# Three reordered steps in a gated attention + two-MoE kernel: POOL's weight sums, one DVE accumulation, one PE reduction

## The chip, the cores and the metric

The kernel runs on one core of a Trainium2 chip. The metric is the device time of one execution in microseconds. Engines are named as the profile names them: PE (matmuls), PEld (its weight loads), DVE (VectorE), ACT (ScalarE), POOL (GpSimd), SP (the queue that issues all DMAs here).

## What is computed

The reference has three stages, each feeding the next:

```python
for t in range(S):                                   # gated linear attention, B=2, H=8, S=768, D=48
    state = alpha[:, :, t, :, None] * state + einsum('bhd,bhe->bhde', k[:, :, t], v[:, :, t])
    y[:, :, t] = einsum('bhd,bhde->bhe', q[:, :, t], state)
x = y as 1536 tokens x 384
xn = x / sqrt(mean(x * x) + 1e-6) * rms_g            # first MoE: 384 -> 1536 -> 384
x  = (silu(xn @ w_gate) * (xn @ w_val)) @ w_out
p  = domain_probs / (sum(domain_probs) + 1e-9)       # second MoE: 4 experts, 384 -> 1024 -> 384
out = sum over e of p[:, e] * (relu(x @ w1[e]) @ w2[e])
```

All is fp32. Each product is made of three matmuls over split operands: a "high" half, rounded, and a "low" half, the rest of it: high x high, high x low, low x high.

## The kernel before

**First stage (to about 320 us).** The 1536 tokens go in four quarters of 384 (index i in the code). For each quarter, a list of events (`events()`) is walked by every engine in its own queue order. In the first MoE a quarter has 12 blocks of hidden columns (f = 0 to 11), and the events per block are G (gate product on PE, Silu on ACT), V (value product on PE, the multiplication on DVE at L1215, the high half on ACT at L891, the low half on POOL at L680) and O (output product). Between these, the table `AT` inserts the steps of the next quarter's attention and normalisation, at a position 3 x f + sub with sub 0, 1, 2 for G of f + 1, V of f + 1 and O of f. Of the normalisation: N (position 24; DVE adds up the squares, L1161 and L1163), SS (position 26; PE waits for `s_sqsum`, then sums over partitions with a matmul against ones, L1509; ACT makes `rms` from it, L864, which needs another activation table), R (28; DVE refines `rms`, L1171 to L1177), X (30; DVE scales). DVE takes the low half of the very last block itself (L1219), and then splits the finished activations `x2` into halves (`split_block`, L1009), six blocks and later three more.

**Second stage (from about 320 us).** The hidden columns of all experts go in 16 pairs of 128 (NPAIR = 16). Pair 0 (PLAIN = 1) is computed plainly (`hidden_plain`). Pairs 1 to 15 use a fast scheme with 15 products: POOL makes 11 sums of weight blocks (`sum_first`, L699 to L705, and `sum_second`, L710 to L714), rounds them (`sum_upper`, L721), and takes the low halves (`sum_lower`, L726 and L728, `sum_lower_last`, L733, which sets `s_wu`). DVE and ACT make 11 sums of activation blocks once (`split_sum`, L1238, which counts `s_vl` to 11), and these serve all pairs. PE (`sums_and_outputs`) interleaves the 15 products of a pair (L1606 to L1608, banks A to F) with the 12 output tiles of the pair before (`out_tile`, L1370 to L1372), and DVE combines the banks (L1295), splits them into halves (`split_bank`, L1232) and accumulates each output tile (`add_up`, L1246 for pair 0, L1249 for all others).

**What sets the order around the change.** POOL's buffers: the sums are written to `u_sum`, which nothing else uses at that time; the rounded halves `wuh` and `wul` of pair 2 lie where the plain weights of pair 0 and some of the activation sums lay, and so need `s_plain` = 6 and `s_vl` = 11. POOL's own order at this place: low half of block 10 of the last quarter (L680), then `sum_weights(2)`, then `out_weights(1)` (L674, L676), then `sum_weights(3)`. `sum_first(pair)` of pairs 3 and on waits for the 15 products of the pair before last (`s_mul`). PE waits for `s_wu` = pair before the first product of a pair. On SP, the load of pair 3's first weights waits for `s_wu` = 1, that of pair 2's second weights for pair 1's `out_weights`.

PE's `out_tile` of tile number n (12 per pair) waits for `s_acc` of n - 1, as two banks alternate; tiles 4 and on of a pair need all six banks split (`s_el`). After pair 15's products PE does tiles 9, 10, 11 of pair 14 and tiles 0 to 11 of pair 15, and each finished tile goes out with a DMA (SP).

Of the kernel before, what the change touches and what calls it, by code (L numbers as in the profile page):

```python
# [26 lines left out]
def gated_attention_two_moe(nc, q, k, v, alpha, w_gate, w_val, w_out, rms_g, probs, w1, w2, out):  # L27
    B, H, S, D = q.shape
    DM, FF = w_gate.shape
    E, _, F2 = w1.shape  # L30
    N = B * S
    NP = H // 2
# [11 lines left out]
    with ctx:  # L44
        def sem(name):
            return ctx.enter_context(nc.semaphore(name))
# [99 lines left out]
        NPAIR, PLAIN = E * F2T // 2, 1  # L146
# [12 lines left out]
        V_SUMS = (0, 1, 2, 3, 4, 5, 7, 9, 10, 13, 14)  # L159
# [24 lines left out]
        def nth(order, q, what):  # L184
            return len(order) * q + order.index(what) + 1
# [90 lines left out]
        s_vs, s_vd, s_vh, s_vl = sem("s_vs"), sem("s_vd"), sem("s_vh"), sem("s_vl")  # L276
        s_plain = sem("s_plain")
# [100 lines left out]
        def raw_1(pair):  # L378
            at = pair % 2 * KT * FW
            return stage[:, :, :].rearrange("p a b -> p (a b)")[:, at:at + KT * FW].rearrange("p (j n) -> p j n", j=KT)  # L380
# [11 lines left out]
        STEP = 6  # L392
        PLACES = (("Y", 6), ("T", 0), ("TQ", 1), ("S", 4), ("KV", 5))
        AT = {}
# [3 lines left out]
        for place in AT.values():  # L398
            place.sort(key=lambda step: step[0] != "Y")
        AT[STEP * NP].append(("N", 0))  # L400
        AT.setdefault(STEP * NP + 2, []).append(("SS", 0))
        AT.setdefault(STEP * NP + 4, []).append(("R", 0))
        AT.setdefault(STEP * NP + 6, []).append(("X", 0))
        AT.setdefault(3 * (FT - 2) + 1, []).append(("XS", 0))
# [209 lines left out]
        def _(pool):  # L614
# [70 lines left out]
            def weight_sums(pair):  # L685
                w = {b: both[pair % 2] for b, both in W.items()}
                return w, {m: u_sum[:, n, :] for n, m in enumerate(U_SUMS)}, 3 * (pair - PLAIN)

            def sum_first(pair):
                w, u, _ = weight_sums(pair)  # L690
                if pair == PLAIN + 1:
                    pool.wait_ge(s_vl, len(V_SUMS))
                    pool.wait_ge(s_plain, 6 * PLAIN)
                elif pair > PLAIN + 1:
                    pool.wait_ge(s_mul, 15 * (pair - PLAIN - 1))
                if pair > PLAIN:
                    pool.wait_ge(s_wu, pair - PLAIN)
                pool.wait_ge(s_r1[pair % 2], 16 * (pair // 2 + 1))
                pool.tensor_tensor(u[12], w[1, 1], w[1, 0], ALU.subtract)  # L699
                pool.tensor_tensor(u[8], w[0, 1], w[0, 2], ALU.subtract)  # L700
                pool.tensor_tensor(u[2], w[1, 0], w[0, 0], ALU.subtract)
                pool.tensor_tensor(u[3], w[0, 0], w[0, 2], ALU.add)
                pool.tensor_tensor(u[4], w[0, 0], w[1, 2], ALU.add)
                pool.tensor_tensor(u[10], w[1, 2], w[0, 2], ALU.subtract)
                pool.tensor_tensor(u[11], w[1, 0], w[1, 2], ALU.add).then_inc(s_us, 1)  # L705
# [9 lines left out]

            def sum_upper(pair):
                c, raw, done = pair % 2, raw_1(pair), 3 * (pair - PLAIN)
                pool.wait_ge(s_us, done + 3)
                for rows, src in ((slice(0, NSUM), u_sum), (slice(NSUM, NSUM + 2), raw[:, 0:2, 0:P]),
                                  (slice(NSUM + 2, NU), raw[:, 1:3, P:FW])):  # L720
                    pool.tensor_scalar(wuh[c][:, rows, :], src, 0.0, 1.0, ALU.add, ALU.mult).then_inc(s_uh, 1)  # L721
# [14 lines left out]
            def sum_weights(pair):  # L736
                sum_first(pair)
                sum_second(pair)
                sum_upper(pair)
                sum_lower(pair)  # L740
                sum_lower_last(pair)
# [254 lines left out]
        def _(dve):  # L996
# [232 lines left out]
            def split_hidden(bank, pair, n, f, t):  # L1229
                at = slice(t * TB3, (t + 1) * TB3)  # L1230
                dve.wait_ge(s_eh, 6 * pair + n + 1)
                dve.scalar_tensor_tensor(out=hidl[pair % 2][:, f, at], in0=bank, scalar=0.0,  # L1232
                                         in1=hidh[pair % 2][:, f, at].bitcast(F32), op0=ALU.max, op1=ALU.subtract
                                         ).then_inc(s_el, 1)
# [5 lines left out]
            def add_up(pair, t):  # L1240
                a = acc[:, t * DM:(t + 1) * DM]
                part = full[f"out_ps{t % 2}"][:, 0:DM]
                p = prob_flat[:, t * E + pair // (F2T // 2):t * E + pair // (F2T // 2) + 1]
                dve.wait_ge(s_tile, NTILE * pair + t + 1)
                if pair == 0:
                    dve.tensor_scalar(a, part, p, None, ALU.mult).then_inc(s_acc, 1)  # L1246
                else:
                    dve.wait_ge(s_acc, NTILE * (pair - 1) + t + 1)
                    dve.scalar_tensor_tensor(out=a, in0=part, scalar=p, in1=a, op0=ALU.mult, op1=ALU.add  # L1249
                                             ).then_inc(s_acc, 1)  # L1250
# [40 lines left out]
            for pair in range(PLAIN, NPAIR):  # L1291
                q = pair - PLAIN

                def combine(bank, part, op):
                    dve.tensor_tensor(bank, bank, tcp[part], op).then_inc(s_add, 1)  # L1295

                def split_bank(bank, f, t):
                    split_hidden(full_bank[bank], pair, BANKS.index(bank), f, t)

                dve.wait_ge(s_mul, nth(MULS, q, 13))  # L1300
                dve.wait_ge(s_copy, nth(COPIES, q, 1))
                combine(bank_f, 1, ALU.subtract)
                add_up(pair - 1, 3)
                dve.wait_ge(s_add, nth(ADDS, q, 7))
                dve.wait_ge(s_copy, nth(COPIES, q, 2))
                combine(bank_f, 2, ALU.subtract)
                add_up(pair - 1, 4)
                dve.wait_ge(s_mul, nth(MULS, q, 4))
                dve.wait_ge(s_copy, nth(COPIES, q, 4))
                combine(bank_d, 4, ALU.subtract)  # L1310
                split_bank("F", 1, 2)
                dve.wait_ge(s_mul, nth(MULS, q, 11))
                dve.wait_ge(s_copy, nth(COPIES, q, 8))
                combine(bank_a, 8, ALU.subtract)
                add_up(pair - 1, 5)
                dve.wait_ge(s_mul, nth(MULS, q, 10))
                dve.wait_ge(s_copy, nth(COPIES, q, 7))
                combine(bank_e, 7, ALU.subtract)
                add_up(pair - 1, 6)
                split_bank("A", 1, 0)  # L1320
                add_up(pair - 1, 7)
                dve.wait_ge(s_mul, nth(MULS, q, 2))
                combine(bank_d, 8, ALU.add)
                dve.wait_ge(s_mul, nth(MULS, q, 9))
                combine(bank_c, 0, ALU.subtract)
                dve.wait_ge(s_add, nth(ADDS, q, 3))
                dve.wait_ge(s_copy, nth(COPIES, q, 3))
                combine(bank_c, 3, ALU.subtract)
                split_bank("E", 0, 0)
                add_up(pair - 1, 8)  # L1330
                split_bank("C", 0, 2)
                dve.wait_ge(s_mul, nth(MULS, q, 5))
                dve.wait_ge(s_copy, nth(COPIES, q, 5))
                combine(bank_b, 6, ALU.subtract)
                if pair == NPAIR - 1:
                    add_up(pair - 1, 9)
                dve.wait_ge(s_add, nth(ADDS, q, 8))
                combine(bank_d, 5, ALU.add)
                if pair < NPAIR - 1:
                    add_up(pair - 1, 9)  # L1340
                add_up(pair - 1, 10)
                dve.wait_ge(s_add, nth(ADDS, q, 1))
                dve.wait_ge(s_copy, nth(COPIES, q, 9))
                combine(bank_b, 9, ALU.subtract)
                if pair == NPAIR - 1:
                    add_up(pair - 1, 11)
                split_bank("D", 1, 1)
                if pair < NPAIR - 1:
                    add_up(pair - 1, 11)
                split_bank("B", 0, 1)  # L1350
                add_up(pair, 0)
                add_up(pair, 1)
                add_up(pair, 2)
            for t in range(3, NTILE):
# [3 lines left out]
        def _(pe):  # L1358
# [52 lines left out]
            for name, i, f in events():  # L1411
# [8 lines left out]
                if name in ("T", "TK", "TQ", "AHEAD", "S", "KV", "Y"):  # L1420
                    n = PAIR_ORDER[f]
                    _, k_dm, q_dm, k_sm, sc_sb, banks, y_bank = own_of(i, f)
# [270 lines left out]
```

## Time and profile before

| | |
|---|---|
| median of 3 runs | 701.38 us (701.12 to 702.0) |
| profiled execution: its own time | 698.92 us |
| profiled execution: span, first to last instruction | 697.2 us |
| granted PE clock | 1.000 over the span |
| PE busy | 683.6 us, 98% |
| DVE, POOL, ACT busy | 466.2 us, 329.1 us, 265.3 us |

The profiled execution is 2.5 us below the median of the others; 1.7 us of its own time lie outside the span. A line of the timeline reads: start in us, duration in us, engine, line, operation, out<-in, shape, count if several were merged; in square brackets the time that the engine stood idle before it and who ended that. Matmuls are pipelined, so a matmul of 384 columns "lasts" 0.33 us but the next starts about 0.17 us later, and one of 512 columns about 0.23 us later.

### The profile page before, as it was taken

What the parts mean: (1) busy time and instruction counts of PE and PEld (TensorE: products, weight loads), DVE (VectorE), ACT (ScalarE), POOL (GpSimd) and SP (SyncE); (2) the same over time, 40 slices, a digit from 0 to 9 for tenths busy, and PEclk for the clock granted to TensorE, in tenths of its full rate; (3) what the DMA queues carried; (4) which work ended last, traced back from release to release, by engine and by line L of the source; (5) the groups of instructions that cost most, each with busy time, mean ns of one, the idle gap of its engine ahead of it and who ended that gap; (6) DMA issues with size and microseconds to landing.
All of it is one profiled execution on the core that took longest, in us unless ns stands there. A gap on an engine that the chain in (4) does not pass through costs nothing.

```text
span 697.2 us, 10727 instructions
## 1 busy us (share of the span) xinstructions
PE 683.6 (98%) x3989; PEld 633.9 (91%) x3989; DVE 466.2 (67%) x819; ACT 265.3 (38%) x482; POOL 329.1 (47%) x416
## 2 busy tenths in 40 slices
PE   7899999999999999999989999999999999999998
PEld 6699999999999999998979999999999999999997
DVE  6876657555556543216968777977797778767875
ACT  3932333222522243227534343433344334443430
POOL 3469761111111115770396586457645775577200
PEclk9999999999999999999999999999999999999999
DMA  8995380005102001000011100111011101100003
GB/s 183 225 182 116 98 170 0 9 1 103 35 1 77 1 2 44 3 0 24 1 46 46 47 23 24 46 46 38 9 46 45 46 2 46 46 24 1 23 1 136
DMA packets 71749, 35.14 MB, mean 50 GB/s; under 512 B 53904, under 2 KB 70672, under 8 KB 71696
## 3 DMA queue, kind: packets, MB, share of 16 engines
q1 hardware_dynamic: 71696, 34.44, 19.6%
q8 instruction: 32, 0.52, 0.3%
q14 instruction: 21, 0.17, 0.1%
HBM read 31.48 MB, written 2.36 MB: 49 GB/s over the span
## 4 chain that ended last, share of the span: by engine, by line
PE 88%; DVE 4%; SPq 3%; POOL 2%; ACT 1%; issue 1%; DMA 1%; DVEq 0%; POOLq 0%
PE out_ps L1370 12%; PE out_ps L1372 12%; PE out_ps L1371 12%; PE hid_ps L1363 7%; PE hid_ps L1365 6%; PE hid_ps L1364 6%; PE at_ps L1608 4%; PE at_ps L1607 4%; PE at_ps L1606 4%; PE hid_ps L1607 2%; PE hid_ps L1608 2%; PE hid_ps L1606 2%; SPq L460 2%; PE at_ps L1444 2%; PE at_ps L1458 1%; PE at_ps L1490 1%
## 5 line engine op out<-in xcount | busy, mean ns | idle before, releaser
L1249 DVE SCALAR_TENSOR_TENSOR x<-out_ps,prob,x 128x384 f32<-128x384 f32 x180 | 110.3, 613 | 58.2 <-PE out_ps L1372 58.2
L1371 PE MATMUL out_ps<-early_r,late_r 128*128 128x384 f32 x384 | 129.4, 337 | 0.0
L1370 PE MATMUL out_ps<-early_r,late_r 128*128 128x384 f32 x384 | 129.0, 336 | 0.4 <-DVE x L1249 0.4
L1372 PE MATMUL out_ps<-early_r,late_r 128*128 128x384 f32 x384 | 129.3, 337 | 0.0
L680 POOL TENSOR_TENSOR hid_lo<-act_sb,hid_hi 128x384 fp32r<-128x384 f32 x44 | 44.9, 1020 | 160.9 <-ACT hid_hi L891 160.9
L941 ACT COPY late<-at_ps 128x512 f32<-128x512 f32 x105 | 61.9, 589 | 103.8 <-PE at_ps L1608 100.8
L1215 DVE TENSOR_TENSOR act_sb<-hid_ps,act_sb 128x384 f32<-128x384 f32 x48 | 26.6, 555 | 79.6 <-PE hid_ps L1365 70.2
L1370 PEld LDWEIGHTS out_ps<-early_r,late_r 128*128 128x128 f32 x384 | 72.1, 188 | 6.6 <-DVE x L1249 0.9
L1371 PEld LDWEIGHTS out_ps<-early_r,late_r 128*128 128x128 f32 x384 | 72.0, 188 | 5.6
L1372 PEld LDWEIGHTS out_ps<-early_r,late_r 128*128 128x128 f32 x384 | 72.1, 188 | 0.0
L699 POOL TENSOR_TENSOR early<-stage 128x128 f32<-128x128 f32 x15 | 7.0, 470 | 126.4 <-PE at_ps L1608 98.8
L891 ACT CAST hid_hi<-act_sb 128x384 fp32r<-128x384 f32 x48 | 24.6, 513 | 107.6 <-DVE act_sb L1215 107.6
L1606 PE MATMUL at_ps<-late_r,early_r 128*128 128x512 f32 x135 | 52.5, 389 | 1.8 <-POOL early_r L733 1.8
L1608 PE MATMUL at_ps<-late_r,early_r 128*128 128x512 f32 x135 | 53.6, 397 | 0.0
L1295 DVE TENSOR_TENSOR at_ps<-at_ps,late 128x512 f32<-128x512 f32 x75 | 52.2, 696 | 0.5
L1363 PE MATMUL hid_ps<-xn_hi,wvh 128*128 128x384 f32 x141 | 49.3, 349 | 0.6 <-POOL wvl L610 0.5
L733 POOL TENSOR_TENSOR early_r<-early,early_r 128x1408 fp32r<-128x1408 f32 x15 | 48.5, 3231 | 0.0
L1607 PE MATMUL at_ps<-late_r,early_r 128*128 128x512 f32 x120 | 47.3, 394 | 0.0
L1365 PE MATMUL hid_ps<-xn_hi,wvl 128*128 128x384 f32 x141 | 47.3, 335 | 0.0
L1364 PE MATMUL hid_ps<-xn_lo,wvh 128*128 128x384 f32 x141 | 47.2, 335 | 0.0
L1370 PE MATMUL out_ps<-hid_hi,woh 128*128 128x384 f32 x132 | 46.4, 351 | 0.0
L1363 PE MATMUL hid_ps<-xn_hi,wgh 128*128 128x384 f32 x132 | 46.1, 349 | 0.2 <-DVE act_sb L1202 0.2
(286 smaller groups left out, 1621.5 us busy)
## 6 DMA issues: line engine op xcount, KB each, us to landing
stage<-in_moe_w_dram SPq DMA_DIRECT2D x32, 384.0 KB, 3.5
alpha_all<-in_alpha_dram SPq DMA_DIRECT2D x8, 288.0 KB, 6.2
stage<-in_moe_w_out_dram SPq DMA_DIRECT2D x4, 576.0 KB, 4.0
out_dram<-x SPq DMA_DIRECT2D x12, 192.0 KB, 1.9
stage<-in_moe_w_gate_dram SPq DMA_DIRECT2D x8, 216.0 KB, 3.9
stage<-in_moe_w_val_dram SPq DMA_DIRECT2D x8, 216.0 KB, 4.0
a_tm<-in_alpha_dram SPq DMA_DIRECT2D x9, 192.0 KB, 4.2
k_tm<-in_k_dram SPq DMA_DIRECT2D x9, 192.0 KB, 3.7
```

The source lines that it names most:

```text
L941: act.copy(tcp[n], bank).then_inc(s_copy, 1)
L1249: dve.scalar_tensor_tensor(out=a, in0=part, scalar=p, in1=a, op0=ALU.mult, op1=ALU.add).then_inc(s_acc, 1)
L1295: dve.tensor_tensor(bank, bank, tcp[part], op).then_inc(s_add, 1)
L1363: pe.matmul(dst, ah, bh, start=(n == 0), stop=False)
L1364: pe.matmul(dst, ah, bl, start=False, stop=False)
L1365: mm = pe.matmul(dst, al, bh, start=False, stop=(n == last))
L1370: pe.matmul(dst, ah, bh, start=first, stop=False)
L1371: pe.matmul(dst, ah, bl, start=False, stop=False)
L1372: return pe.matmul(dst, al, bh, start=False, stop=last)
L1606: pe.matmul(bank, ah, bh, start=first, stop=False, skip_group_check=True)
L1607: pe.matmul(bank, ah, bl, start=False, stop=False, skip_group_check=True)
L1608: pe.matmul(bank, al, bh, start=False, stop=True, skip_group_check=True).then_inc(s_mul, 1)
```

## The change

Three things move; no instruction is added and none is taken away.

- The SS event goes from position 26 to 27, so on PE the matmul of L1509 comes after the gate product of block 10 and not before it; on ACT `rms` comes after that block's Silu. It applies to the SS of quarters 1 to 3.
- The two waits of pair 2 (`s_vl`, `s_plain`) go from the start of `sum_first` to the start of `sum_upper`. POOL may make pair 2's 11 sums as soon as it is through with pair 1's and block 10.
- In the last pair, DVE accumulates tile 0 (`add_up(15, 0)`) between the split of bank D and the split of bank B, no longer after both.

```diff
-        AT.setdefault(STEP * NP + 2, []).append(("SS", 0))
+        AT.setdefault(STEP * NP + 3, []).append(("SS", 0))
...
             def sum_first(pair):
                 w, u, _ = weight_sums(pair)
-                if pair == PLAIN + 1:
-                    pool.wait_ge(s_vl, len(V_SUMS))
-                    pool.wait_ge(s_plain, 6 * PLAIN)
-                elif pair > PLAIN + 1:
+                if pair > PLAIN + 1:
                     pool.wait_ge(s_mul, 15 * (pair - PLAIN - 1))
...
             def sum_upper(pair):
                 c, raw, done = pair % 2, raw_1(pair), 3 * (pair - PLAIN)
+                if pair == PLAIN + 1:
+                    pool.wait_ge(s_plain, 6 * PLAIN)
+                    pool.wait_ge(s_vl, len(V_SUMS))
                 pool.wait_ge(s_us, done + 3)
...
                 split_bank("D", 1, 1)
                 if pair < NPAIR - 1:
                     add_up(pair - 1, 11)
+                else:
+                    add_up(pair, 0)
                 split_bank("B", 0, 1)
-                add_up(pair, 0)
+                if pair < NPAIR - 1:
+                    add_up(pair, 0)
                 add_up(pair, 1)
```

## Rows read from the trace of the kernel before

**Rows 1.** The page: the chain that ended last, shares by engine.

```profile
PE 88%; DVE 4%; SPq 3%; POOL 2%; ACT 1%; issue 1%; DMA 1%; DVEq 0%; POOLq 0%
```

**Rows 2.** PE's waits over the whole span: us in total, times, longest; the top line.

```profile
PE at_ps L1606 <- POOL early_r L733: 1.8, 1, 1.8
```

**Rows 3.** Timeline of PE, at the start of pair 2.

```profile
352.52 0.40 PE L1608 MATMUL at_ps<-late_r,early_r 128*128 128x512 f32 x1
354.76 0.49 PE L1606 MATMUL at_ps<-late_r,early_r 128*128 128x512 f32 x1 [1.84 <-POOL early_r L733]
355.09 0.39 PE L1607 MATMUL at_ps<-late_r,early_r 128*128 128x512 f32 x1
```

**Rows 4.** Timeline of POOL, from the last low half on, and two later pairs.

```profile
314.24 1.02 POOL L680 TENSOR_TENSOR hid_lo<-act_sb,hid_hi 128x384 fp32r<-128x384 f32 x1 [0.46 <-ACT hid_hi L891]
342.88 0.47 POOL L699 TENSOR_TENSOR early<-stage 128x128 f32<-128x128 f32 x1 [27.62 <-DVE late_r L1238]
...
347.90 1.39 POOL L721 TENSOR_SCALAR early_r<-early 128x1408 fp32r<-128x1408 f32 x1
...
351.51 3.20 POOL L733 TENSOR_TENSOR early_r<-early,early_r 128x1408 fp32r<-128x1408 f32 x1
...
378.16 0.47 POOL L699 TENSOR_TENSOR early<-stage 128x128 f32<-128x128 f32 x1 [6.12 <-PE at_ps L1608]
...
401.19 0.47 POOL L699 TENSOR_TENSOR early<-stage 128x128 f32<-128x128 f32 x1 [8.42 <-PE at_ps L1608]
```

**Rows 5.** Timeline of DVE, from the last low half to pair 1.

```profile
318.87 0.56 DVE L1219 TENSOR_TENSOR hid_lo<-act_sb,hid_hi 128x384 fp32r<-128x384 f32 x1 [0.58 <-ACT hid_hi L891]
319.39 3.70 DVE L1009 TENSOR_TENSOR late_r<-x,late_r 128x512 fp32r<-128x512 f32 x6
323.85 1.90 DVE L1009 TENSOR_TENSOR late_r<-x,late_r 128x512 fp32r<-128x512 f32 x3 [0.76 <-ACT late_r L909]
...
343.84 0.69 DVE L1295 TENSOR_TENSOR out_ps<-out_ps,late 128x512 f32<-128x512 f32 x1
```

**Rows 6.** Timeline of PE, from the first stage into pair 0.

```profile
320.07 0.68 PE L1399 MATMUL out_ps<-hid_lo,woh 128*128 128x384 f32 x3
320.59 0.39 PE L1370 MATMUL at_ps<-late_r,early_r 128*128 128x512 f32 x1
```

**Rows 7.** Timelines of POOL and of DVE at 100 us.

```profile
99.86 1.02 POOL L610 TENSOR_TENSOR wol<-stage,woh 128x384 fp32r<-128x384 f32 x1
...
100.01 1.29 DVE L1161 TENSOR_TENSOR x_nrm<-x_nrm 128x384 f32<-128x384 f32 x1 [2.47 <-ACT x_nrm L804]
101.33 0.56 DVE L1163 TENSOR_TENSOR x_nrm<-x_nrm 128x384 f32<-128x384 f32 x1
```

**Rows 8.** Timelines of PE at 101 us, of ACT and DVE at 180 us.

```profile
101.38 0.34 PE L1372 MATMUL out_ps<-hid_hi,wol 128*128 128x384 f32 x1
101.94 0.91 PE L1509 MATMUL at_ps<-x_nrm,ones 128*128 128x384 f32 x2 [0.23 <-DVE x_nrm L1163]
...
179.08 0.58 ACT L864 ACTIVATE rms<-at_ps,consts 128x384 f32<-128x384 f32 x1
179.68 1.28 ACT L885 ACT_TABLE_LOAD   x1
...
181.50 0.56 DVE L1215 TENSOR_TENSOR act_sb<-hid_ps,act_sb 128x384 f32<-128x384 f32 x1 [3.42 <-ACT act_sb L885]
```

**Rows 9.** Timelines of DVE and of PE after the last pair's products.

```profile
681.61 0.68 DVE L1232 SCALAR_TENSOR_TENSOR late_r<-hid_ps,late_r 128x512 fp32r<-128x512 f32 x1
682.21 0.68 DVE L1232 SCALAR_TENSOR_TENSOR late_r<-at_ps,late_r 128x512 fp32r<-128x512 f32 x1
682.81 1.13 DVE L1249 SCALAR_TENSOR_TENSOR x<-out_ps,prob,x 128x384 f32<-128x384 f32 x2
...
682.75 0.34 PE L1372 MATMUL out_ps<-early_r,late_r 128*128 128x384 f32 x1
683.47 0.44 PE L1370 MATMUL out_ps<-early_r,late_r 128*128 128x384 f32 x1 [0.39 <-DVE x L1249]
```

## The prediction, made before the changed kernel was run

> **What bounds the kernel now.** I read the chain that ended last first: PE holds 88% of it [rows 1], so the kernel is a row of matmuls in PE's queue order, and only what stops PE, or what comes after its last matmul, is worth time. The second view is therefore PE's own waits. Its top line, and the largest wait of PE in the whole span, is one wait for POOL's L733, 1.8 us [rows 2]. The next ones after 100 us are small: 0.39 us for DVE's L1249 in the tail [rows 9], 0.23 us for DVE's L1163 at 102 us [rows 8]. The third view is the timeline of each of these three places, with the releasing engine beside PE. The three parts of the change touch exactly one place each. Everything else PE does between them is back to back, and a microsecond won at a place travels to the end unchanged as long as nothing else becomes late on the way.
>
> What the waits view calls 1.8 us is not the price. Matmuls overlap, so I count from start to start. At the beginning of pair 2 the last product of pair 1 starts at 352.52 and the first of pair 2 at 354.76: 2.24 us, where 0.23 is usual, so 2.01 us; the one after it starts 0.33 us later (355.09), another 0.10 above the usual [rows 3]. Together 2.11 us.
>
> **Part 1, POOL's sums of pair 2.** Before, POOL is through with block 10's low half at about 315.2 (the row says 314.24 + 1.02 and such an instruction is followed after 0.97), then stands for 27.62 us until DVE's last activation sum, and starts the sums at 342.88. The 11 sums take until the first rounding at 347.90, which is 5.02 us; the last low half ends at 351.51 + 3.20 = 354.71 [rows 4], and PE starts 0.05 us later [rows 3]. With the change the sums run from 315.2 to about 320.2, in the time POOL stood idle: they need pair 1's weights finished (before 314.24, as POOL works in order) and the raw weights of pair 2, loaded long before. At 342.88 POOL starts with the rounding. All that follows is 5.02 us earlier and the weights are ready at 349.7. PE asks for them at 352.52 + 0.23 = 352.75: 3.06 us of margin. The wait goes as a whole, -2.11 us. What is late next? The second weights of pair 1 and the raw loads that SP issues on those semaphores also come 5 us earlier. Pair 3's sums then wait for the last product of pair 1 (about 353) and start earlier than before too. In the later pairs POOL waits 8.42 us for PE before each round, and the round comes every 23.03 us [rows 4], so POOL has nothing to give there and nothing to lose.
>
> The cost of this part lies at its new place. Where POOL reads SBUF with two inputs while DVE does the same, the trace shows them one after the other: at 100.01 DVE's addition takes 1.29 us, its like right after it 0.56 us, and it ends 0.42 us after the end of POOL's instruction at 99.86 + 1.02 = 100.88 [rows 7]. DVE's operations with one input in PSUM don't show it: the one at 343.84 ran beside POOL's sums and took 0.69 us, the usual for its kind [rows 4, 5]. The sums that move come to lie beside two-input work of DVE: the low half at 318.87 and the six splits from 319.39, 0.6 us each [rows 5]. I step through it. By 318.87, eight sums have started, the ninth (the others being 0.42 to 0.55 apart) runs until 319.15. The low half then ends at about 319.6, not 319.43; PE needs it at 320.07 [rows 6]; hidden. Two sums are left. If the engines take turns, the tenth runs to 320.0, the first split to 320.55, the eleventh to 320.95, the second split to 321.5. PE starts pair 0's first product at 320.59 and the next block of it 0.7 us later [rows 6]; the first split used to be ready at about 320.0 and is now ready just at the start, the second about 0.15 us after PE wants it. With the start-up of a matmul after a wait, 0.1 us as above, I take 0.35 us. The ends: 0 if DVE gets in first each time and the two sums run after it; 0.9 us if POOL keeps going to 320.2 with all its sums (splits 1.1 us later, of which 0.5 us of PE's lead over them takes its share, plus the restarts). DVE is then up to 0.8 us late in a stretch in which it works without a break to 343, but a 0.76 us wait for ACT's L909 sits in it at 323.85 [rows 5] and takes nearly all of that; and the margin of 3.06 us covers the rest.
>
> This is also where a page bears on the change. The Trainium skill, "SBUF — State Buffer", section "Who interferes with whom", says that a DVE instruction with two SBUF inputs contends with a GpSimd instruction that reads SBUF, that whoever issues first has the shared pair for the whole instruction, and that a DVE instruction with at most one SBUF input does not contend. The trace agrees on both (1.29 against 0.56 us, and the undisturbed 0.69 us). By this rule the part costs between nothing and the turn-taking above; it speaks against moving the sums beside DVE's splits, but not by enough to cancel 2.11 us.
>
> **Part 2, SS one step later.** At quarter 1 the matmul against ones starts 0.56 us after the last one of O (101.38 to 101.94), where 0.17 is usual: 0.39 us lost [rows 8], because DVE's x_nrm sum was held up by POOL and ended only at 101.89 [rows 7]. One gate product is 9 x 0.17 = 1.55 us of PE work that needs none of this, so the new place comes at 101.55 + 1.55 = 103.1, 1.2 us after the operand. -0.39 us. At quarters 2 and 3 PE does not wait there and nothing is won; the matmul itself, and the slow start of the product behind it, move along and cost the same. ACT's `rms` comes later: at quarter 2 it starts at 179.08 before and, by the queue order of Silu 0.49, table load 1.28, then rms, at about 180.7 after, done at 181.3. It is asked for by DVE's L1171, behind the multiplication of 181.50, which today waits for ACT because two table loads of 1.28 us stand before its Silu [rows 8]. With the change that Silu is early, the multiplication starts with PE's value product, and `rms` is there when it ends. So nothing later than before, cost zero; if this cover failed, DVE's refinement would start some tenths later with PE's next use of it several us away.
>
> **Part 3, the tail.** Pair 15's tile 2 needs the accumulation of tile 0. PE's matmul of 682.75 is followed at 683.47: 0.72 less 0.17 is 0.55 us lost. DVE's accumulation stands behind the two splits of 681.61 and 682.21 and starts at 682.81, ends at about 683.42, and PE starts 0.05 later [rows 9]. Tile 0 was complete at about 682.0, so with the change the accumulation takes the place of the second split: 682.21 to 682.82. PE's natural time is 682.92. That is 0.1 us of margin, just enough or just too little for the weight load before it, so of the 0.55 and the restart of 0.1 that the changed spacing also holds, I take 0.55. The split of bank B ends 0.5 us later, at 683.4; it is needed by tile 4, which cannot start before 685. The accumulation of tile 1 starts where it did. What is late next is tile 3 behind tile 1's accumulation (ends 683.94, wanted at 684.0): a tenth at most.
>
> **The sum.** -2.11 + 0.35 - 0.39 - 0.55 = -2.70 us. The profiled span would go from 697.2 to 694.5, its own time from 698.92 to 696.2. The runs' median is 701.38, 2.5 us above the profiled execution; the terms are fixed amounts, not shares, so I take them off the median: 698.7 us.
>
> **Rivals.**
> (a) POOL keeps the port: all sums go through before DVE's splits, 0.9 us instead of 0.35. Result 699.2. For it: DVE waited its whole turn at 100.01. Against: it waited for one instruction, and POOL has to wait for its own earlier sums twice in the eleven.
> (b) Parts 2 and 3 bring nothing, because the margins of 0.1 us in the tail fail or the 0.39 comes back as another wait in the next steps of quarter 1. Result 701.38 - 1.76 = 699.6. For it: the thin margin. Against: the 1.2 us of margin at SS.
> (c) The change doesn't do what it says: PE no longer waits for POOL at 352.75, but then for DVE or ACT, which today have 2 us of rest there. Up to 2.11 is gone: 701.38 - 0.59 = 700.8. Against: the same order of work runs in every later pair at 23.03 us without a wait of PE.
> (d) Slower. PE in pairs 3 to 15 runs in lockstep with POOL, DVE and ACT; shifting POOL by 5 us at pair 2 could leave them in a phase where each pair has a small stall. 13 pairs, so it decides from 2.70 / 13 = 0.21 us a pair; 0.3 us would give 701.38 - 2.70 + 3.9 = 702.6. Against: POOL is released by PE in each pair after 8.42 us of rest [rows 4], and found its rhythm within one pair even after the 2.11 us hole.
>
> **How the numbers follow.** Forecast 0.66, (a) 0.12, (b) 0.10, (c) 0.09, (d) 0.03. A measurement of this kernel can tell about 0.2%, 1.4 us, from no change. Faster by more than that is the forecast, (a) and most of (b): 0.87; within it (c) and a rest of (b): 0.10; slower 0.03. The range: at the low end the collision costs nothing and the tail gives its restart too, 701.38 - 3.16 = 698.2, less 0.6 for the scatter of the runs shown (702.0 - 701.38), 697.6. At the high end (b) with the same scatter, 700.2, and a tenth more: 700.3.
>
> **What would show it.** Pair 2's first matmul starts 0.23 us after the last of pair 1, POOL's L733 for pair 2 ends some 3 us before it, and POOL's sums stand between 315 and 321. DVE's L1009 splits at 319 to 323 are stretched or spaced by up to 0.5 us, and PE shows a wait for them of 0.1 to 0.5 us at 320 to 322: if there is none, that term was too dear. No wait before L1509 at 103. In the tail the gap of 0.72 is down to 0.2 or 0.3. Wrong would be a new wait of PE on DVE or ACT after pair 2's first product, or a pair that takes more than 23.03 us from one L699 to the next.

## The result, and the profile after

| | before | after |
|---|---|---|
| median | 701.12 us (5 runs, 699.0 to 702.0) | 696.48 us (5 runs, 695.44 to 697.87) |
| ratio | | 0.9942, 95% interval 0.9918 to 0.9966 |
| profiled execution: own time, span | 698.92, 697.2 us | 695.44, 693.7 us |
| granted PE clock, mean | 1.000 | 0.998 |

The kernel became faster, by 4.6 us between the medians; I had forecast 2.7, to 698.7 us, and a range that ends at 697.6. The direction was right, the size and the range were not. The time fell outside my range on the low side, by 1.1 us. Between the two profiled executions it is 3.5 us.

The page of after: busy times and the chain by engine, where PE went from 88% [rows 1] to 92% and POOL from 2% to 1%.

```profile
PE 683.7 (99%) x3989; PEld 634.2 (91%) x3989; DVE 466.7 (67%) x819; ACT 265.3 (38%) x482; POOL 329.1 (47%) x416
...
PE 92%; SPq 3%; DVE 1%; DMA 1%; ACT 1%; POOL 1%; issue 1%; DVEq 0%
```

PE is busy for the same 683.7 us: nothing was taken out but holes. Line numbers have moved in two places: POOL's sums stand three lines higher (L699 to L714 of before are L696 to L711 here), and everything on PE from L1350 on three lines lower, so L1606 of before is L1609 here; L721 and L733 are unchanged. The timeline of PE at the start of pair 2, then POOL's for the weights it needs:

```profile
351.76 0.40 PE L1611 MATMUL at_ps<-late_r,early_r 128*128 128x512 f32 x1
352.00 0.39 PE L1609 MATMUL at_ps<-late_r,early_r 128*128 128x512 f32 x1
...
314.24 0.47 POOL L696 TENSOR_TENSOR early<-stage 128x128 f32<-128x128 f32 x1
...
317.73 0.46 POOL L708 TENSOR_TENSOR early<-early,stage 128x128 f32<-128x128 f32 x1
318.27 0.66 POOL L710 TENSOR_TENSOR early<-early,stage 128x128 f32<-128x128 f32 x1
318.89 0.90 POOL L711 TENSOR_TENSOR early<-early,stage 128x128 f32<-128x128 f32 x1
342.19 1.38 POOL L721 TENSOR_SCALAR early_r<-early 128x1408 fp32r<-128x1408 f32 x1 [22.39 <-DVE late_r L1238]
...
345.78 3.24 POOL L733 TENSOR_TENSOR early_r<-early,early_r 128x1408 fp32r<-128x1408 f32 x1
```

The 2.24 us from matmul to matmul [rows 3] are 0.24. The last low half ends at 349.02, 2.98 us before PE asks (predicted 3.06). The last two sums are stretched, from 0.46 to 0.66 and 0.90 us; that is the collision with DVE, which e4 below puts to the test. DVE and PE at that place, which answer to [rows 5, 6]:

```profile
317.90 0.70 DVE L1219 TENSOR_TENSOR hid_lo<-act_sb,hid_hi 128x384 fp32r<-128x384 f32 x1 [0.58 <-ACT hid_hi L891]
318.53 6.25 DVE L1009 TENSOR_TENSOR late_r<-x,late_r 128x512 fp32r<-128x512 f32 x9
...
319.62 0.48 PE L1373 MATMUL at_ps<-late_r,early_r 128*128 128x512 f32 x1
319.94 0.39 PE L1374 MATMUL at_ps<-late_r,early_r 128*128 128x512 f32 x1
...
320.40 0.49 PE L1373 MATMUL at_ps<-late_r,early_r 128*128 128x512 f32 x1
320.73 0.39 PE L1374 MATMUL at_ps<-late_r,early_r 128*128 128x512 f32 x1
```

DVE's nine splits now run as one block of 6.25 us, and the wait of 0.76 us for ACT that stood between the sixth and the seventh [rows 5] is gone in it. On PE the second matmuls of the first two blocks start 0.32 and 0.33 us after the first ones where 0.23 is usual, 0.19 us together.

SS (against [rows 8]): the matmul against ones follows the gate product at once, 0.18 us after the matmul before it. The pair of such matmuls is also 0.10 us shorter, 0.81 against 0.91 us, which matters below. At quarter 2 `rms` ends at 180.27, and DVE asks for it at 180.66:

```profile
102.47 0.34 PE L1368 MATMUL hid_ps<-xn_hi,wgl 128*128 128x384 f32 x1
102.65 0.81 PE L1512 MATMUL at_ps<-x_nrm,ones 128*128 128x384 f32 x2
...
179.69 0.58 ACT L864 ACTIVATE rms<-at_ps,consts 128x384 f32<-128x384 f32 x1
...
180.19 0.56 DVE L1215 TENSOR_TENSOR act_sb<-hid_ps,act_sb 128x384 f32<-128x384 f32 x1 [3.08 <-PE hid_ps L1368]
180.66 0.56 DVE L1171 SCALAR_TENSOR_TENSOR at_ps<-at_ps,rms 128x384 f32<-128x384 f32 x1
```

The tail (against [rows 9]): the accumulation stands between the two splits, and 0.72 us on PE have become 0.18, with 0.22 behind it:

```profile
678.73 0.68 DVE L1232 SCALAR_TENSOR_TENSOR late_r<-hid_ps,late_r 128x512 fp32r<-128x512 f32 x1
679.33 0.61 DVE L1249 SCALAR_TENSOR_TENSOR x<-out_ps,prob,x 128x384 f32<-128x384 f32 x1
679.85 0.68 DVE L1232 SCALAR_TENSOR_TENSOR late_r<-at_ps,late_r 128x512 fp32r<-128x512 f32 x1
...
679.87 0.34 PE L1375 MATMUL out_ps<-early_r,late_r 128*128 128x384 f32 x1
680.05 0.39 PE L1373 MATMUL out_ps<-early_r,late_r 128*128 128x384 f32 x1
680.27 0.33 PE L1374 MATMUL out_ps<-early_r,late_r 128*128 128x384 f32 x1
```

So each part did what it says. The open question was one of size: in these two traces the three places make 3.0 us, and the medians 4.6.

### The profile page after: what moved, and what is told of

It reads as the page before. It is cut to its first block, busy times and chain, and to the rows that moved or that the text cites. A ratio compares the mean times of both kernels' runs of the same rounds, so it can differ in the third digit from the quotient of the medians.

```text
span 693.7 us, 10727 instructions
## 1 busy us (share of the span) xinstructions
PE 683.7 (99%) x3989; PEld 634.2 (91%) x3989; DVE 466.7 (67%) x819; ACT 265.3 (38%) x482; POOL 329.1 (47%) x416
## 4 chain that ended last, share of the span: by engine, by line
PE 92%; SPq 3%; DVE 1%; DMA 1%; ACT 1%; POOL 1%; issue 1%; DVEq 0%
PE out_ps L1373 13%; PE out_ps L1375 13%; PE out_ps L1374 13%; PE hid_ps L1366 7%; PE hid_ps L1368 6%; PE hid_ps L1367 6%; PE at_ps L1611 5%; PE at_ps L1610 5%; PE at_ps L1609 4%; PE hid_ps L1610 2%; PE hid_ps L1611 2%; PE hid_ps L1609 2%; SPq L460 2%; PE at_ps L1447 2%; PE at_ps L1461 1%; PE at_ps L1493 1%
## 5 line engine op out<-in xcount | busy, mean ns | idle before, releaser
L696 POOL TENSOR_TENSOR early<-stage 128x128 f32<-128x128 f32 x15 | 7.0, 464 | 101.7 <-PE at_ps L1611 101.7
L1609 PE MATMUL at_ps<-late_r,early_r 128*128 128x512 f32 x135 | 52.4, 388 | 0.0
L733 POOL TENSOR_TENSOR early_r<-early,early_r 128x1408 fp32r<-128x1408 f32 x15 | 48.5, 3235 | 0.0
```

The costliest lines, as they stand in the source:

```text
L1609: pe.matmul(bank, ah, bh, start=first, stop=False, skip_group_check=True)
```

## The experiments

**How they are compared.** The times of single executions of one kernel spread over 1 to 5 us, more than most terms. The traces repeat far better once they are cut at the same matmuls. Four stretches, each from the start of one PE matmul to that of another, in us, cover the three places: (S) O of block 8 to O of block 11 in the first quarter, with SS in it; (C) pair 0's first product to its first output tile, with the collision; (H) from there to the last pair's first output tile, with pair 2's hole; (T) from there to the last matmul.

| kernel | S | C | H | T |
|---|---|---|---|---|
| before | 12.98 | 13.65 | 346.48 | 13.19 |
| after | 12.50 | 13.86 | 344.36 | 12.57 |
| e1_again | 12.50 | 13.82 | 344.36 | 12.68 |
| e2_null | 12.95 | 13.64 | 348.00 | 13.16 |
| e3_pool_only | 12.93 | 13.86 | 344.36 | 13.17 |
| e4_half | 12.50 | 13.64 | 344.36 | 12.69 |
| e5_filled | 12.95 | 13.65 | 348.39 | 13.22 |
| e6_longer | 12.98 | 13.64 | 349.65 | 13.21 |
| e7_ss_only | 12.50 | 13.64 | 348.02 | 13.20 |
| e8_tail_only | 12.94 | 13.65 | 346.46 | 12.68 |
| e9_filled9 | 12.92 | 13.64 | 346.50 | 13.16 |
| e10_collide | 12.50 | 14.02 | 344.36 | 12.70 |
| e11_null2 | 12.95 | 13.64 | 346.49 | 13.20 |
| e12_null3 | 12.96 | 13.64 | 346.48 | 13.14 |
| e13_null4 | 12.94 | 13.64 | 346.47 | 13.21 |
| e14_null5 | 12.94 | 13.64 | 346.47 | 13.20 |
| e15_longer2 | 12.93 | 13.64 | 349.64 | 13.17 |

**The change again, and the kernel before again.** No edit; both on the chip of e3 and e4.

> The changed kernel once more, beside the kernel before on one chip. Theory A (the priced terms are the whole effect: -2.11 pair 2, +0.19 collision, -0.49 at SS, about -0.6 tail, sum about -3.0 us, and the rest of the -4.64 us between the medians is the scatter of executions, which already spans 699.0 to 702.0 us for the kernel before): ratio near 0.9957, difference 2.5 to 3.6 us. Theory B (the change takes away something that the one profiled execution of before did not show, worth 1.5 us more): ratio near 0.994 again, difference over 4 us, and the first products of the first stage come at other times than in the kernel before.

Ratio 0.9951, interval 0.9937 to 0.9966: 3.4 us (2.4 to 4.4). The middle of it lies in theory A's range of 2.5 to 3.6, and the interval reaches into that of B. All four stretches repeat those of after to 0.11 us. What differs is the start: the output product of its block 3 comes 1.7 us later than in the profiled run of after (65.83 against 64.09), and its span is 1.9 us longer, nearly all of it from there. PE's waits between 44 and 60 us name the larger part of it, 1.5 us for POOL where after had 0.3, most of it for weight pieces of the first MoE:

```profile
PE hid_ps L1366 <- POOL wvl L610: 0.7, 1, 0.7
PE hid_ps L1366 <- POOL wgl L610: 0.5, 1, 0.5
PE out_ps L1373 <- POOL hid_lo L680: 0.3, 1, 0.3
```

> The kernel before, unchanged, as a run of its own: how far two sets of the same program lie apart. Theory A: ratio 1.000 within 0.002, and its profile differs from the earlier profile of the kernel before only up to about 60 us (the first products of the first stage start some tenths of a us earlier or later); from there to pair 2 and through the tail the intervals are the same to 0.1 us, the wait of 1.8 us for POOL among them. Theory B: the intervals after 60 us differ too, by 0.5 us or more, so that the profiled execution of before was not typical.

Ratio 1.0006 (0.9996 to 1.0015), the two sets of one program agree, as A wants. But its trace does not: stretch H is 1.52 us longer than in the first profile of the same program, with the same wait of 1.8 us for POOL in it. Theory A is wrong on that; it is what B had asked for, an interval after 60 us that differs by over 0.5 us, though B had no cause for it. The view by stretches shows where: of 355 to 360 us the granted clock is 0.66 (PEclk, the third number from the right), and PE's timeline shows the matmuls of 384 columns start every 0.32 us instead of 0.17, right behind the hole:

```profile
355.00:360.00 5.00, 5.00 (x19) 4.74 (x20) 1.20 (x3) 1.08 (x2) 4.92 (x9) 0.66 0.26 83
...
354.84 0.49 PE L1606 MATMUL at_ps<-late_r,early_r 128*128 128x512 f32 x1 [1.80 <-POOL early_r L733]
...
355.82 0.47 PE L1371 MATMUL out_ps<-early_r,late_r 128*128 128x384 f32 x1
356.09 0.52 PE L1372 MATMUL out_ps<-early_r,late_r 128*128 128x384 f32 x1
356.41 0.52 PE L1370 MATMUL out_ps<-early_r,late_r 128*128 128x384 f32 x1
...
358.97 0.48 PE L1372 MATMUL out_ps<-early_r,late_r 128*128 128x384 f32 x1
359.28 0.39 PE L1606 MATMUL out_ps<-late_r,early_r 128*128 128x512 f32 x1
```

From 355.9 to 359.3, 1.0 us behind the end of the hole, the array had its lower level, 1.2 instead of 2.4 GHz. The trace of before on which I predicted had full clock here. This made a new theory (C): the hole costs its 2.11 us always, and in a part of the executions another 1.5 us of clock. Its rival (D): the half clock falls where it likes.

**POOL's part alone.** The diff of `sum_first` and `sum_upper`, without the other two.

> Only POOL's sums of pair 2 ahead of the two waits; SS and the tail as before. Theory A: PE's hole of 2.11 us at pair 2 is gone, 0.19 us come at the start of pair 0's plain product: -1.9 us, ratio 0.9973. Theory B (the three parts together gave more than their terms, and this one is the large one): -3 us or more.

H is 344.36, 2.12 us less, and C 0.21 more, as theory A has it to 0.02 us; S and T stay. By time it is 0.9963 (0.9949 to 0.9977), -2.6 us, which is more than the 1.9 of the terms and leaves both open.

**Seven of eleven sums ahead.** The waits stand at the start of `sum_second`.

```diff
             def sum_second(pair):
                 w, u, done = weight_sums(pair)
+                if pair == PLAIN + 1:
+                    pool.wait_ge(s_plain, 6 * PLAIN)
+                    pool.wait_ge(s_vl, len(V_SUMS))
                 pool.wait_ge(s_us, done + 1)
```

> The changed kernel, but only the first seven sums of pair 2 go ahead of the waits; the last four come after them. The seven end before DVE's two-input work begins. Theory A (port collision of two-input work on DVE and POOL): DVE's low half back at 0.56 us and its splits at 0.60 us each, no slow starts of PE at pair 0's first two blocks, so 0.19 us less than the changed kernel; POOL's weights of pair 2 ready 1.9 us later than in the changed kernel (four sums), still 1.1 us before PE asks. Rival (the stretch of DVE comes from ACT's casts at the same time, not from POOL): DVE's durations stay at 0.70 and 0.95 us.

All as theory A says. DVE is back at its old durations, with ACT's casts beside it as before, so these were not the cause:

```profile
318.06 0.56 DVE L1219 TENSOR_TENSOR hid_lo<-act_sb,hid_hi 128x384 fp32r<-128x384 f32 x1 [0.58 <-ACT hid_hi L891]
318.59 3.70 DVE L1009 TENSOR_TENSOR late_r<-x,late_r 128x512 fp32r<-128x512 f32 x6
```

C is 13.64, that of before, and H 344.36, that of after: the collision's 0.2 us are saved and nothing is lost, because the last low half, at 347.67 + 3.25 = 350.92 in this run, still comes over a microsecond early. Ratio 0.9954 (0.9940 to 0.9969), median 696.28. It is the best version here by its trace; the times cannot tell 0.2 us from the change.

**More sums beside DVE's work.** Four extra sums of pair 2, written to places that are overwritten later, ahead of the eleven, in the changed kernel.

```diff
+                if pair == PLAIN + 1:
+                    for m in (0, 1, 6, 7):
+                        pool.tensor_tensor(u[m], w[0, 1], w[0, 2], ALU.subtract)
                 pool.tensor_tensor(u[12], w[1, 1], w[1, 0], ALU.subtract)
```

> The changed kernel with four more sums of pair 2 on POOL ahead of the eleven (into places that are overwritten later), so that six and not two of POOL's two-input additions meet DVE's low half and splits. Theory A (they take turns, one instruction each): the splits of 0.60 us become 0.95 us each for five or six in a row, and PE's first blocks of pair 0 wait 0.3 to 0.7 us in sum where the changed kernel loses 0.19. Rival (POOL keeps going with all it has): DVE's low half ends 2 us late and PE waits for it already at the last output product.

Neither is quite it. DVE's low half waits through three of POOL's sums in a row and takes 1.47 us; only where POOL stops for its own semaphore, at 319.6, does DVE get in, and from there the two take turns:

```profile
318.60 1.47 DVE L1222 TENSOR_TENSOR hid_lo<-act_sb,hid_hi 128x384 fp32r<-128x384 f32 x1 [0.58 <-ACT hid_hi L894]
...
318.74 0.49 POOL L704 TENSOR_TENSOR early<-stage 128x128 f32<-128x128 f32 x1
319.16 0.48 POOL L705 TENSOR_TENSOR early<-stage 128x128 f32<-128x128 f32 x1
319.73 0.65 POOL L710 TENSOR_TENSOR early<-early,stage 128x128 f32<-128x128 f32 x1
320.34 0.90 POOL L711 TENSOR_TENSOR early<-early,stage 128x128 f32<-128x128 f32 x1
```

PE already waits in the last output product, and the slow or late starts from there to the third block add up to 1.1 us against 0.19 in the changed kernel. (Part of it falls ahead of stretch C, which grows by only 0.37 us over before.) So the price of this place is steep: four sums of 0.43 us more, 0.9 us more on PE.

**SS alone, the tail alone.** The one line of `AT`; the five lines around `split_bank("B", 0, 1)`.

> Only SS one step later. Theory A: the interval from O6's to O33's first matmul in quarter 0's walk is 0.49 us shorter than in the kernel before (54.38 us there, 53.95 in the changed kernel), the hole at pair 2 and the tail as before; -0.4 to -0.5 us, which the times can hardly tell. Rival (it only works together with the others): no such shortening.

From the output product of block 2 to that of block 11 it is 53.92 us, 0.46 less than in before; S is 12.50 as in after, C and T as before. Ratio 0.9987 (0.9973 to 1.0002). Its H is 348.02: it has the hole, and its granted clock is at half from 354.5 on for 3.4 us.

> Only the last pair's first accumulation ahead of bank B's split. Theory A: from the first output tile of the last pair to the last matmul 12.6 us instead of 13.19, everything else as in the kernel before, -0.6 us. Rival: the wait turns up at the next tile (tile 3 on tile 1's accumulation) and the stretch stays at 13.1 to 13.2.

T is 12.68, 0.5 us less, and no wait turns up at the next tile. Ratio 0.9996 (0.9981 to 1.0011), too coarse to see it.

**The hole filled.** PE's queue gets matmuls of ones against ones into the free bank A ahead of its wait for pair 2's weights, in the kernel before. In the first version 18 of them, in the second 9.

```diff
+                if q == 1:
+                    bank_free("A")
+                    for _ in range(9):
+                        pe.matmul(bank_a[:, 0:P], ones[:, :], ones[:, :], start=True, stop=True)
                 pe.wait_ge(s_wu, q + 1)
```

> The kernel before, and in PE's wait for pair 2's weights 18 matmuls of ones against ones into the free bank A, so that PE works through the hole while it waits just as long. Theory C (the hole of 2.1 us costs more than itself: in some executions the granted clock falls to half for 3.4 us right behind it, as at 355.9 us in the run of the kernel before at 0.995, which is worth 1.5 us there): no half clock after 300 us, no execution with a mean clock of 0.995 for that reason, and a mean time 0.3 to 0.7 us below the kernel before, although no wait is shorter. Theory D (the half clock at 355.9 was chance, and the change is worth its terms, 3.0 us): same time and same clocks as the kernel before within 0.2 us.

I had mis-sized it: each of the 18 goes in two passes of 0.11 us, 4.0 us in all, so H grew to 348.39, by 1.91. The times rose by 1.3 us between the means (701.26 for 12 executions, 699.92 for 33 of the kernel before), 0.6 less than that. There is no half clock behind pair 2 in the trace. But 4 of these 12 executions have a mean clock of 0.995, as low as with two half-clock stretches, against 7 of 33 at 0.995 or lower in the kernel before: the filling did not make low clocks rarer. Weak for C, and no clean test.

> As the filled hole, but with 9 matmuls of ones (18 passes of 0.11 us, 2.0 us in all) and not 18, which had taken 4.0 us and so made the stretch 1.9 us longer by itself. PE waits for the same weights at the same time and is busy meanwhile. Theory C: from the first output tile to the last pair 346.4 to 346.6 us, as in the executions of before without a half clock; no half clock behind pair 2; mean time 0.4 to 0.7 us below the kernel before, none of the executions with two half-clock stretches or fewer than before. Theory D: mean time as the kernel before within 0.2 us, half clocks as often.

This time the filling fits, and PE waits for the same weights until the same moment:

```profile
352.68 0.40 PE L1608 MATMUL at_ps<-late_r,early_r 128*128 128x512 f32 x1
352.92 2.17 PE L1619 MATMUL at_ps<-ones 128*128 128x128 f32 x18
354.92 0.50 PE L1606 MATMUL at_ps<-late_r,early_r 128*128 128x512 f32 x1
```

H is 346.50, that of before with full clock, and the clock behind the hole is full; by itself that says little, as most traces with the idle hole have it too. The mean is 699.45 us (12 executions) against 699.93 (17), 0.5 less, with a ratio of 0.9993 (0.9979 to 1.0006): the size that C expects, but not clear of zero. One of the 12 has a mean clock of 0.995, of the 17 five are at or below it, which leans to C as well, on small counts.

**The hole made longer.** The four extra sums of e10, in the kernel before, where they delay pair 2's weights.

> The kernel before with four more sums on POOL ahead of pair 2's (written to places that are overwritten later), so that the hole of PE at pair 2 is 3.8 us and not 2.1. Theory C: the half clock comes behind it in most executions, so +1.7 us for the hole and about +1 us more for the clock: 2.7 us over the kernel before, with a mean clock below 1.0 in nearly all. Theory D: +1.7 us alone, clocks as in the kernel before.

The hole is 3.48 us in the waits view, and the clock falls at its end (half from 356.20 to 359.61), to 0.57 of full in the stretch from 356 to 360:

```profile
356.30 0.80 PE L1609 MATMUL at_ps<-late_r,early_r 128*128 128x512 f32 x1 [3.48 <-POOL early_r L736]
356.89 0.63 PE L1610 MATMUL at_ps<-late_r,early_r 128*128 128x512 f32 x1
...
356.00:360.00 4.00, 3.70 (x12) 3.41 (x12) 0.15 (x1) 1.08 (x2) 3.92 (x6) 0.57 0.00 2
```

H is 349.65, 3.17 more than in before: 1.7 of hole, 1.5 of clock. Ratio 1.0040 (1.0023 to 1.0057), +2.8 us, as C says. Of its ten executions none has a mean clock of 1.0, of 79 of the kernel before 30 have; but of the ten of the changed kernel, which has no hole, only one has, so the mean clock is a poor witness of what follows the hole. The reason is in the traces: 10 of the 17 profiled executions, with and without the hole, have half-clock stretches somewhere between 13 and 31 us too, in the first stage. What those cost was not measured.

**More profiled executions of both.**

> Another look at the kernel before: whether the granted clock is at half right behind the hole of pair 2 (as in two of four looks at kernels with this hole) or not. Theory C expects it about every second time, and then a stretch from the first output tile to the last pair of 348.0 us, otherwise 346.5.

> A further look at the kernel before. Theory C (half clock for 3.4 us right behind the hole of 2.1 us in about two executions of five): either a half clock beginning 1 to 2 us after the end of the hole and 348.0 us from the first output tile to the last pair, or full clock and 346.5 us. A half clock elsewhere in the second stage, away from the hole, speaks for theory D (chance).

> The same, for the count: theory C gives a half clock behind the hole or none in the second stage, theory D one anywhere.

> The same, for the count: theory C gives a half clock behind the hole or none in the second stage, theory D one anywhere.

> A second look at the kernel with the hole of 3.8 us. Theory C: half clock behind it again, the stretch from the first output tile to the last pair 349.6 us; theory D: full clock and 348.1 us, or a half clock somewhere else.

The four of the kernel before have full clock throughout the second stage, H 346.47 to 346.49. The longer hole has the half clock again, from 356.0 on, H 349.64. Together: behind the hole of 2.1 us the clock is at half in 2 of 8 profiled executions (e2 and e7, of before, e2, e7, e8, e11 to e14), behind the one of 3.8 us in 2 of 2, and in 7 profiled executions without an idle hole there (after, e1, e3, e4, e5, e9, e10) never. It begins between 0.1 us before and 1.0 us after the first matmul behind the hole, lasts 3.4 us, and elsewhere in the second stage it is never at half before the last matmul. Four such stretches in the same place out of 375 us are not chance, so D does not hold. C holds in kind; that it is every second time, as I wrote for e11, is too often.

## Why the prediction was right or wrong, point by point

**What bounds the kernel; three places, three terms.** Right. The stretches above give what each was worth (after and e1 against before): pair 2 -2.12 (forecast -2.11), the collision +0.19 (+0.35), SS -0.48 (-0.39), tail -0.56 (-0.55). e3, e7 and e8 show the three parts one by one. Sum -2.97 where the forecast has -2.70; every sign is right, and the largest term is right to 0.01.

**The collision.** The mechanism was the one told from [rows 7], and e4 shows it by taking it away. The size was off because in my stepping the second split came 0.15 us too late for PE, and in the run both blocks started in time and paid only the slow second start, 0.1 us each. Rival (a), that POOL keeps going, did not happen here but is real: e10 shows POOL holding DVE out for three instructions. That it stayed cheap in the change may be luck of the phase: POOL stopped for its own semaphore between the ninth sum, which ends at 318.19, and the tenth, from 318.27, just where DVE wanted in. This is read from two traces and was not tested. The Trainium skill, "SBUF — State Buffer", section "Who interferes with whom", has whoever issues first hold the shared ports for the whole instruction, with the other blocked meanwhile. The traces agree for one instruction against one (POOL's 0.66 and 0.90 us); that a waiting engine can be passed over three times in a row goes beyond it.

**SS.** The term was 0.39 by the start of one matmul; the stretch says 0.42 to 0.48, by the execution. The rest is the restart: of the two matmuls against ones the second started 0.43 us after the first behind the wait, and starts 0.32 us after it without one. That is 0.1 us more, visible as 0.91 [rows 8] against 0.81 us. I had counted such a restart at pair 2 and left it out here.

**The step that failed: the base.** The last step of the sum took -2.70 us off the median of three runs, 701.38 us. Over 79 executions of the kernel before the mean is 699.95 (standard deviation 1.1 us), so 1.4 of the 2.2 us by which the predicted time missed were in the number that I started from; from 699.95 the same sum gives 697.25, within 0.8 of the median. The range allowed 0.6 us for scatter, which is how far the highest of those three runs lay above their median; built on 699.95 the same range would reach down to 696.2 and hold the result. (Its low end adds up to -3.15, not -3.16, which changes nothing.) The profiled execution, 698.92 and 2.5 us below the median, was the hint: I called the difference fixed and took the worse end of it.

**Also too small: the sum of the terms.** It was -2.70 where the three places gave -2.97, by the collision and by the restart at SS. Beyond that I took the hole's 2.01 + 0.10 us "as a whole" from one trace in which the granted clock was full. In executions with the half clock behind it, the same hole costs 3.6 us. At 2 of 8, that is 0.4 us on the mean (an estimate from eight executions, with a wide margin), so -2.97 becomes about -3.35. The means, 699.95 us over 79 executions of the kernel before and 696.60 over the ten of the changed one, differ by 3.35 us with a standard error of 0.3. That fits, but it does not decide: 2.97 is only 1.3 standard errors away, and the mean granted clock is 0.998 in both sets. That the hole can cost 1.5 us of clock is shown by the traces; that this share of the measured difference comes from it is not. I had read the clock, 1.000, as a property of the kernel and not of that execution. The Trainium skill, "TensorE: Matmul & The Clock Gate", Part 1, says that the throttled state is the default and that activity releases it. The traces agree in kind, as the clock went to half behind an idle PE in 4 of 10 profiled executions with a hole; I had not asked of any wait what follows it.

**What is next.** Nothing new was late on PE at pair 2, in the tail, or at SS, and rivals (b), (c) and (d) fall: S is shorter by 0.5 us in e7 and T in e8, and H is 344.36 in all five profiled executions without hole or filling, so PE waits for nobody else at pair 2 and no later pair has a stall.

The 4.6 us between the first medians, against 3.35 between the means, is scatter: the five runs of before in that comparison have a mean of 700.72, and the five of after 696.66. Sources of scatter seen here are the clock and the start: until block 3 of the first quarter, profiled executions of kernels that are the same up to there differ by up to 1.7 us, in good part by when POOL has the first MoE's weight pieces ready.

## What to carry to other kernels

Price a hole on the path by what may follow it as well: look at the granted clock right behind it, in more than one execution, because one trace can show the cheap case. Cut traces at the same instruction and compare stretches; tenths that no timing can tell then repeat to a few hundredths (0.13 us at worst here), and the whole time is taken from many executions and not from three. When work is pulled forward into idle time of POOL, move only as much as the wait needs: the last four of the eleven sums bought nothing and cost 0.2 us beside DVE's two-input work.

## What the runs showed of the hardware

- A hole of 2.1 us on PE was followed by half the granted clock for 3.4 us in 2 of 8 profiled executions, and not in others of the same program; one of 3.8 us in both seen. The cost was 1.5 us each time (H 348.00 and 348.02 against 346.48). The one trace with a hole of 2 us filled by matmuls without use and the one with 4 us of them have full clock, which two traces cannot make a rule.
- POOL additions that follow one another without a wait kept a two-input DVE operation out for three instructions (1.47 us instead of 0.56); after a stop of POOL they took turns. What decides between the two is open.
- A matmul of 128 columns of fp32 ones against ones goes in two passes of 0.11 us each.
